# The compact read of the inverses on ScalarE's DMA queue, and their write at the odd step's end

## What is computed

```python
for t in range(S):
    y[:, :, t] = np.einsum('bhd,bhde->bhe', rt, state)
    Sa = np.einsum('bhde,bhe->bhd', state, at)
    state_decay = state * wt[:, :, None, :] - np.einsum('bhd,bhe->bhde', Sa, bt)
    state = state_decay + np.einsum('bhd,bhe->bhde', vt, kt)
...
solu = h * sm                      # h = x @ w_in, sm = softmax of h
ln = (solu - mu) / np.sqrt(var + 1e-06) * g_ln      # then ln @ w_out
g = np.maximum(h, 0.0) + alpha * np.minimum(h, 0.0) # h = x @ w_in of the second layer, then g @ w_out
```

## Time and profile before

| | us |
|---|---|
| median of 3 runs | 1062.67 |
| lowest, highest | 1058.58, 1063.07 |
| the profiled execution | 1061.18 |
| its span, first to last instruction | 1059.4 |
| attention part, roughly | the first 475 of the span |

### The profile page before, as it was taken

One profiled execution on the slowest core, in us unless ns is written; L12 is line 12 of the kernel. 1 busy time (PEld: TensorE's weight loads), 2 busy tenths in 40 slices (PEclk: granted clock), 3 DMA queues, 4 the chain that ended last, 5 costly groups with the idle time before them and its releaser, 6 DMA issues.

```text
span 1059.4 us, 31704 instructions
## 1 busy us (share of the span) xinstructions
PE 918.4 (87%) x13408; PEld 868.3 (82%) x13408; DVE 625.9 (59%) x1087; ACT 478.8 (45%) x1011; POOL 220.0 (21%) x452
## 2 busy tenths in 40 slices
PE   3479669769769777978899999999999999999998
PEld 3369668668668766867789999999999999999998
DVE  7867446457545644455675665757566475655644
ACT  3345444444544645343663443535344353543533
POOL 8568542442343352100000000000000000000000
PEclk9689889889889889999999999999999999999999
DMA  5636454455356334233401000000000000000000
GB/s 153 145 83 142 111 115 107 112 112 132 87 124 146 103 86 101 64 85 104 145 14 26 1 26 26 1 25 0 25 0 25 25 0 25 0 25 7 7 14 13
DMA packets 144095, 67.35 MB, mean 64 GB/s; under 512 B 118844, under 2 KB 129980, under 8 KB 143980
## 3 DMA queue, kind: packets, MB, share of 16 engines
q1 hardware_dynamic: 143980, 65.66, 25.2%
HBM read 45.98 MB, written 19.66 MB: 62 GB/s over the span
## 4 chain that ended last, share of the span: by engine, by line
PE 62%; DMA 14%; DVE 9%; ACT 7%; issue 5%; SPq 3%; POOL 0%; ACTq 0%; DVEq 0%; POOLq 0%
DMA dc<-d_scr 7%; PE acc L1117 5%; PE px L341 5%; PE acc L1118 5%; PE acc L1119 5%; DMA l_scr<-lb 4%; PE mid L1117 3%; PE mid L1118 3%; PE mid L1119 3%; PE bank L1117 3%; PE bank L1119 3%; PE bank L1118 3%; PE pa L310 3%; DMA d_scr<-s_x 2%; PE pr L365 2%
## 5 line engine op out<-in xcount | busy, mean ns | idle before, releaser
L1383 POOL TENSOR_TENSOR stats<-stats 128x1 f32<-128x1 f32 x24 | 13.2, 551 | 561.0 <-DVE stats L1445 561.0
L1307 ACT ACTIVATE stage<-mid 128x512 f32<-128x512 f32 x96 | 57.1, 595 | 159.2 <-PE mid L1188 159.2
L1470 DVE SCALAR_TENSOR_TENSOR stage<-mid,slopes 128x512 f32<-128x512 f32 x96 | 66.4, 691 | 105.6 <-ACT slopes L1311 105.6
L1117 PE MATMUL acc<-wo_h,act_h 128*128 128x320 f32 x384 | 122.0, 318 | 6.8 <-DVE act_l L1397 6.1
L1118 PE MATMUL acc<-wo_h,act_l 128*128 128x320 f32 x384 | 119.0, 310 | 0.0
L1119 PE MATMUL acc<-wo_l,act_h 128*128 128x320 f32 x384 | 118.6, 309 | 0.0
L1117 PE MATMUL mid<-zT_h,w_h 128*128 128x256 f32 x384 | 108.2, 282 | 4.3 <-DVE zT_l L1397 4.3
L1118 PE MATMUL mid<-zT_h,w_l 128*128 128x256 f32 x384 | 107.7, 280 | 0.0
L1119 PE MATMUL mid<-zT_l,w_h 128*128 128x256 f32 x384 | 107.3, 279 | 0.0
L809 POOL TENSOR_TENSOR al<-al,prod 40x512 f32<-40x512 f32 x48 | 61.0, 1271 | 163.8 <-DMA al<-a_features_first 120.8
L365 PE MATMUL pr<-rhs,hh 64*64 64x40 f32 x768 | 35.0, 259 | 68.8 <-ACT rhs L685 68.8
(11 more groups left out here) (163 smaller groups left out, 2461.8 us busy)
## 6 DMA issues: line engine op xcount, KB each, us to landing
wkb<-wkb_features_first SPq DMA_DIRECT2D x46, 242.5 KB
rvu<-rv_features_first SPq DMA_DIRECT2D x48, 160.0 KB
l_scr<-lb SPq DMA_DIRECT2D x24, 256.0 KB, 4.3
x_scr<-x SPq DMA_DIRECT2D x24, 256.0 KB, 3.7
al<-a_features_first SPq DMA_DIRECT2D x48, 80.0 KB
sv<-v_time_first SPq DMA_DIRECT2D x48, 80.0 KB, 2.8
out<-y_sb SPq DMA_DIRECT2D x11, 320.0 KB, 2.3
d_scr<-s_x SPq DMA_DIRECT2D x12, 256.0 KB, 3.5
```

Source lines behind the costliest of these rows:

```text
L1117: pe.matmul(o, left[0], right[0], start=start, stop=False)
L1307: act.activation(neg[q % 2][:], mid[q % 2][:], ACT.Relu, scale=-1.0).then_inc(neg_ready, 1)
L1470: dve.scalar_tensor_tensor(out=act_f[q % 2][:], in0=mid[q % 2][:], scalar=0.0, in1=slope[q % 2][:], op0=ALU.max, op1=ALU.add).then_inc(act ...
```

## The change

`d_read` moves from SyncE to ScalarE. ScalarE issues it in the prologue ahead of `spread_d(0)`, and in even step n for pair n/2+1 right behind `take_uT(n)`, with its two waits: `dd_ready` (ScalarE's own earlier spread) and `d_out` (the write has landed). `d_write(n // 2 + 1)` leaves the even step n and is issued at the end of the odd step n-1, behind `l_write`. The two edits together also free SyncE of the wait for `d_out`.

```diff
@@ -222,12 +222,6 @@
             sp.dma_start(d_scr[p].rearrange("k l x -> l k x"),
                          s_x[:].rearrange("p k s t -> p k (s t)")).then_inc(d_out[p % 2], 16)
 
-        def d_read(p):
-            wait(sp, dd_ready, NB * p)
-            sp.wait_ge(d_out[p % 2], use(p, 2, 16))
-            blocks = d_scr[p].rearrange("k l x -> (k l) x").rearrange("(l b) (s t) -> (b s) l t", b=2 * NB, t=SB)
-            sp.dma_start(dc[:], blocks).then_inc(d_back[p % 2], 16)
-
         def save_y(m):
             sp.wait_ge(y_stored, m + 1)
             sp.dma_start(x_scr[m], x[m % 2][:].rearrange("p n t -> p (n t)")).then_inc(y_saved[m % 2], 16)
@@ -251,14 +245,12 @@
                 load_rv(m)
             l_write(1)
             d_write(0)
-            d_read(0)
             l_read(1)
             load_a(5)
             load_wkb(5)
             load_a(6)
             load_wkb(6)
             d_write(1)
-            d_read(1)
             load_wkb(7)
             l_write(2)
 
@@ -269,17 +261,12 @@
                 load_v(2)
             if n % 2 == 0 and n + 4 < NG:
                 l_read((n + 4) // 2)
-            inverses = n % 2 == 0 and 0 < n < NG - 2
-            if inverses:
-                d_write(n // 2 + 1)
             if n + 8 < NG:
                 load_wkb(n + 8)
             if n > 0:
                 save_y(n - 1)
             if n + 2 < NG:
                 load_rv(n + 2)
-            if inverses:
-                d_read(n // 2 + 1)
             if n + 3 < NG:
                 load_v(n + 3)
 
@@ -289,6 +276,8 @@
             beside(sp, n)
             if n % 2 == 1 and n + 5 < NG:
                 l_write((n + 5) // 2)
+            if n % 2 == 1 and n + 3 < NG:
+                d_write((n + 3) // 2)
         save_y(NG - 1)
 
     def tensor(pe, beside):
@@ -719,6 +708,12 @@
             for half in range(2):
                 act.copy(a_bd[ER[half], half], al[m % 7][ER[half], half]).then_inc(a_bd_ready, 1)
 
+        def d_read(p):
+            wait(act, dd_ready, NB * p)
+            act.wait_ge(d_out[p % 2], use(p, 2, 16))
+            blocks = d_scr[p].rearrange("k l x -> (k l) x").rearrange("(l b) (s t) -> (b s) l t", b=2 * NB, t=SB)
+            act.dma_start(dc[:], blocks).then_inc(d_back[p % 2], 16)
+
         def spread_d(p):
 
             act.wait_ge(d_back[p % 2], use(p, 2, 16))
@@ -756,6 +751,7 @@
                 if 0 < m < AHEAD - 3:
                     spread_a(m + 1)
                 take_kbn(m)
+            d_read(0)
             act.wait_ge(masks_loaded, 16)
             spread_d(0)
             spread_a(AHEAD - 2)
@@ -768,6 +764,8 @@
             front = n + AHEAD < NG
             take_u(n)
             take_uT(n)
+            if n % 2 == 0 and n + 2 < NG:
+                d_read(n // 2 + 1)
             if 0 < n and n + AHEAD - 1 < NG:
                 take_kbn(n + AHEAD - 1)
             if n == 0:
```

## The result

| | median us | lowest, highest | runs |
|---|---|---|---|
| kernel before | 1059.2 | 1054.5, 1063.9 | 20 |
| changed kernel | 1066.4 | 1055.0, 1076.8 | 20 |

The ratio of changed to before is 1.0042, with a 95% interval of 1.0022 to 1.0063: 4.4 us slower, within the 0.5% that I had set as no change (the interval reaches a little beyond it), and far from the 51 us gained that were forecast. The medians of this table lie further apart, by 7.2 us, since the changed kernel's runs spread more widely. The spans of the two profiled executions are 1064.5 and 1059.4 us, so the traces show the same 5 us.

What follows compares the result with a forecast made beforehand. The prediction took the chain of waits over the attention part, led by the compact read, as the bound. 36 + 4 + 13.5 - 2 = 51.5 us off 1061.2 gave 1009.7, forecast as 1011 us, range 985 to 1045.

Steps and rivals of the forecast that it cites:

- Part 1, the write: Odd step's end: inverses' write goes out right behind the block write, landing at 296.1 in step 12 (295.5 to 297.4).
- Part 2, ScalarE's issue and stall: Even steps: ScalarE's issue under 1 us, its wait about 2.1 us; scores at most 0.3 to 0.6 us late, costing nothing.
- rivals that held ScalarE in the issue: Even steps: ScalarE held while others' transfers drain; 1096 us (chance 0.05), or 1062 us with a cancelling gain (0.05).
- the write in its queue: Even steps: inverses' write lands late, near 299.3, each step gaining about 1 us; 1052 us, chance 0.05.
- Part 2, the issue 3.7 us earlier: Even steps: compact read's issue moves from 299.94 to about 296.2 in step 12, 3.7 us earlier (2.5 to 4.4).
- Part 2, the landing: Nine even steps: read lands earlier, gains of 2.2 to 6.4 us possible; 4.0 us taken for each, 36 us.
- last of everything again: Slow end for the even steps' read: it lands at 306.1 in step 12, a gain of 2.2 us.
- first rival: Even steps: read issued 3.7 us earlier but landing as slowly as before, clock falling every time; 1027 us, chance 0.22.
- Step 20: Even step without a block write: read no longer waits behind the x save, spread 4.4 us earlier, 4 us taken.
- Start-up: First compact read now has other loads beside it: 0 to 4.4 us more, 2 us taken as lost.
- The clock: Odd steps: shorter idle time keeps TensorE's clock high in 5 of 9, 2.7 us each, 13.5 us gained.
- a gain that just cancels: Even steps: ScalarE partly held in the read's issue, offset by an equal gain; 1062 us, chance 0.05.

Runs made afterwards that it cites:

- dose table: Read on ScalarE, SyncE's loads held until it lands: 1009.4 us; against that, weights let through 1030.3 us, weights, x save and r/v let through 1043.5 us.
- small decoy: Useless 256 KB copy in 4096 pieces added on SyncE's queue, against the kernel with the read on ScalarE and SyncE's loads held: 1020.1 us.
- 1003 us kernel: Compact read on SyncE moved ahead of the lane read too, against the kernel with the early write and read on SyncE (1014 us): 1002.7 us.

## Why the prediction was wrong, point by point

- **What bounds the kernel** was right: with the round trip of the inverses shortened, the kernel gains 4.7 to 5.6% (1014 to 1003 us).
- **Part 1, the write.** Right. Its landing in step 12 is 6.33 us behind the block write's issue (309.91 - 303.58); I had 6.05 (296.1 - 290.05). The upper bound was 7.35.
- **Part 2, ScalarE's issue and stall.** Right. The issue took 0.37 us, and the stall delayed the scores by little. ScalarE's timeline in step 12, answering to rows 6:

```profile
309.99 0.37 ACTq L715 DMA_DIRECT2D dc<-d_scr  x1
310.45 0.75 ACT L700 COPY kbn<-pa 128x320 f32<-128x320 f32 x2 [2.83 <-DMA d_scr<-s_x]
```

TensorE's timeline there, answering to rows 7:

```profile
312.58 1.09 PE L299 MATMUL pa<-a_bd,wkb 128*64 128x128 f32 x16 [0.43 <-issue]
...
315.77 1.13 PE L344 MATMUL pr<-sv,al 128*64 128x40 f32 x32
...
323.16 1.93 PE L354 MATMUL pr<-rhs,hh 64*64 64x40 f32 x32 [5.35 <-ACT rhs L674]
```

The scores start 9.29 us into the step (312.58 - 303.29), where they stood 8.60 us in before (298.36 - 289.76): 0.7 us late, and I had at most 0.6; the right-hand side ends at 316.90 and waits for the read, as said. The rivals that held ScalarE in the issue or the write in its queue did not come.
- **Part 2, the issue 3.7 us earlier.** Nearly: 3.0 on average of nine (9.8 to 6.8).
- **Part 2, the landing: the step that failed.** I took the gain of 4.0 us a step from a landing a little faster than before, and as the slow end of the term a read that comes "last of everything again", 9.9 us after its issue. The mean came out at 10.3, with 13.2 in step 14: worse than my slow end, which I had treated as an end and not as the likely case. (The middle of my two cases is 304.0, not the 304.2 that I wrote; nothing hangs on it.) Two things were wrong. A read in its own queue does not overtake the other queue's transfers; each group of them that was let through beside it made it later, also those issued after it (the dose table). And the budget of 9.2 us of engine time was read from a stretch in which SyncE was held behind the read, so it lacked the transfers that the change sets free: from the read's issue to its landing alone the records now add up to 9.4 us of engine time in step 12 (8.39 x 1.12) and 11.5 in step 14 (13.21 x 0.87). A mean over 16 engines also hides how long the last pieces wait on the busiest of them; that is my inference from step 14's 1491 late records. Stretches after, columns as in rows 8 (the DMA share is the number behind the granted clock), from the read's issue to its landing in step 12, in step 14 and at start-up. In the two even steps the DMA share is 1.12 (above 1, so the records overlap; I read it as full) and 0.87, more than the 0.71 that I used; at start-up it is no higher than the 0.82 of before, but at 149 GB/s instead of 79, since most of it is other transfers:

```profile
309.99:318.38 8.39, 7.40 (x252) 6.69 (x248) 3.72 (x6) 2.41 (x5) 5.16 (x11) 1.00 1.12 180
345.57:358.78 13.21, 7.59 (x244) 6.69 (x240) 3.27 (x6) 2.41 (x5) 10.29 (x29) 0.97 0.87 179
43.10:54.14 11.04, 0.00 (x0) 0.00 (x0) 6.53 (x7) 0.00 (x0) 7.66 (x14) 0.50 0.77 149
```

- **The first rival** (1027 us, "lands as slowly as before") had the right direction and too small a size. The Trainium skill's sentence that a second issuer saves only issue time ("DMA: Bandwidth & Descriptors", "Issuing engines are not separate DMA queues") would have been the better guide, and even it was too kind: here the move to the second queue made a read land 3.4 us later. The Trainium skill says on the same page, in the section "Queues, rings and completion order", that a DMA engine goes round between the queues that have work, packet by packet. By that rule a read in many small packets ends behind a queue with few large ones, which the dose table agrees with. The small decoy tests it only in part, since most of the read was out before the decoy moved; what it shows is not against the rule.
- **Step 20:** 4.0 us forecast, 4.0 measured.
- **Start-up:** the sign was right, the size not: 2 us forecast, 7.7 measured (11.04 against 4.11 us of landing), beyond my end of 4.4. This term is of the same kind as the main one and was mis-sized for the same reason.
- **The clock:** 13.5 us forecast, 1.3 measured over nine odd steps (16.0 to 15.8). With the stall hardly shorter there was little to save. But the term was wrong for a shorter stall too: I took it that five of the nine would keep the clock after 2.4 to 5.7 us of idle time, and in the 1003 us kernel, with 1.2 to 3.0 us of it, only two of nine odd steps did. The last section has more.
- **Chances.** The case "a gain that just cancels" had 0.05, and its number came (1062 against 1066), but not its mechanism: ScalarE was not held in the issue. No rival had the read landing later than before in step after step, though the trace held its parts: SyncE's 7.41 us of held loads behind the read were a sign of what the change would set free beside it.

## What to carry to other kernels

In this kernel a transfer in small pieces on the critical path was not delayed by what stood behind it in its own queue (5.2 us with all loads there, 5.3 with 4096 pieces more), and was delayed by what another queue moved beside it (5.9 to 10.3 us). So before moving a blocking DMA to another engine, list what the old queue will now issue during its flight, and budget the DMA engines with that in; then hold those loads, or put the transfer first in the shared queue. And where a wait can be shortened by order alone, try order first: write and read moved up within one queue gave 60 us here, the second queue without a hold none, and with one 53.

## What the runs showed of the hardware beyond that

Short stalls did not protect TensorE's clock here. In the 1003 us kernel the nine odd steps follow stalls of 1.18 to 2.98 us (idle ahead of the solve). Two of them had a granted clock of 1.00, behind 1.70 and 1.94 us; in the other seven it was at the lower of its two levels for a time, 0.79 to 0.90 in the mean. The length of the last stall alone does not tell which: step 9 follows 1.70 us and step 15 only 1.18. Stretches of this kernel, columns as in rows 8, step 9 and step 15:

```profile
208.36:222.10 13.74, 13.74 (x397) 12.78 (x397) 11.51 (x20) 7.98 (x21) 11.70 (x27) 1.00 0.55 163
302.69:319.97 17.28, 15.46 (x396) 14.34 (x397) 12.07 (x20) 8.81 (x23) 14.93 (x31) 0.90 0.50 140
```

TensorE's timeline at the start of each, with the idle time ahead in the bracket. Step 15 has another 0.58 us of it shortly before, with which the two come to about the same, 1.76 and 1.70 us:

```profile
208.36 1.13 PE L365 MATMUL pr<-rhs,hh 64*64 64x40 f32 x32 [1.70 <-ACT rhs L685]
...
300.42 0.32 PE L429 MATMUL py<-q,kbn 128*40 128x64 f32 x4 [0.58 <-issue]
...
302.69 1.81 PE L365 MATMUL pr<-rhs,hh 64*64 64x40 f32 x32 [1.18 <-ACT rhs L685]
```

Over the nine odd steps this kernel saved 0.7 us each against before (16.0 to 15.3), where I had put 2.7 for five of nine. The odd step at 302.69 also holds 1.82 us of idle time that no wait explains, so not all of its 17.28 us is the clock's.
